# Second layer of a retention-and-MoE kernel: from eight block products to Strassen's seven

## The reference

```python
scores = scale * np.matmul(q, k.transpose(0, 1, 3, 2))   # 4 batches, 8 heads, 576 tokens, 64 dims
x = np.matmul(scores * Dmat, v)                          # decayed causal mask
h = x @ w_in                                             # first layer, 512 -> 2048
g = np.where(h >= 1, h, np.where(h <= -1, 0, (h + 1) ** 2 / 4))
x = g @ w_out                                            # 2048 -> 512
a, b = x @ w_a, x @ w_b                                  # second layer, 512 -> 1536 twice
out = (a * b) @ w_out2                                   # 1536 -> 512
```

## Time and profile before

| | |
|---|---|
| median of three runs | 913.02 us |
| the profiled execution | 915.21 us |
| its span in the trace | 912.7 us |
| TensorE busy | 902.3 us, 99% |
| VectorE, ScalarE busy | 348.2 us, 285.0 us |
| second layer on TensorE | from 462.3 us to 908.3 us |

### The profile page before, as it was taken

The page is one execution under the profiler, slowest core; times in us unless marked ns, Lnnn a source line. Parts: engine busy times, 40 slices in busy tenths (PEclk is TensorE's granted clock), DMA queues, the critical chain, the costliest instruction groups (busy, mean ns, idle before and its releaser), DMA issues.

```text
span 912.7 us, 12087 instructions
## 1 busy us (share of the span) xinstructions
PE 902.3 (99%) x5160; PEld 766.0 (84%) x5160; DVE 348.2 (38%) x565; ACT 285.0 (31%) x476; POOL 36.7 (4%) x54
## 2 busy tenths in 40 slices
PE   7999999999999999999999999999999999999998
PEld 6998888888899888888888888888899888888886
DVE  4686655434445433546653213111222311131112
ACT  1245454333445333535542112111211211121111
POOL 4550000000000000000000000000000000000000
PEclk9999999999999999999999999999999999999999
DMA  9996000000000000013330000100010000010001
GB/s 344 313 357 236 1 0 1 1 1 1 1 1 1 1 1 1 1 69 105 104 104 1 0 1 10 38 1 0 1 47 2 24 0 1 1 47 0 1 1 46
DMA packets 20053, 42.46 MB, mean 47 GB/s; under 512 B 1568, under 2 KB 12320, under 8 KB 20000
## 3 DMA queue, kind: packets, MB, share of 16 engines
q1 hardware_dynamic: 19856, 41.50, 13.1%
q10 hardware_dynamic: 144, 0.20, 0.1%
HBM read 36.97 MB, written 4.72 MB: 46 GB/s over the span
## 4 chain that ended last, share of the span: by engine, by line
PE 98%; DMA 1%; DVE 0%; ACT 0%; POOL 0%; issue 0%; SPq 0%; POOLq 0%
PE score_b L386 5%; PE score_a L386 5%; PE score_b L385 5%; PE score_a L385 5%; PE score_a L384 5%; PE score_b L384 5%; PE score_a L332 4%; PE kv_b L349 4%; PE score_a L333 4%; PE kv_b L350 4%; PE score_b L333 4%; PE score_a L334 4%; PE ret_b L350 4%; PE score_b L332 4%; PE ret_b L349 4%; PE ret_b L351 4%
## 5 line engine op out<-in xcount | busy, mean ns | idle before, releaser
L501 DVE TENSOR_TENSOR gate_w<-relu_s,relu_r 128x512 f32<-128x512 f32 (+1 forms) x80 | 51.1, 639 | 131.6 <-ACT relu_r L613 131.6
L385 PE MATMUL score_b<-xl,w_all 128*128 128x512 f32 (+1 forms) x240 | 88.3, 368 | 0.0
L386 PE MATMUL score_b<-xh,w_all 128*128 128x512 f32 (+1 forms) x240 | 88.3, 368 | 0.0
L385 PE MATMUL score_a<-xl,w_all 128*128 128x512 f32 (+1 forms) x240 | 88.3, 368 | 0.0
L386 PE MATMUL score_a<-xh,w_all 128*128 128x512 f32 (+1 forms) x240 | 88.3, 368 | 0.0
L384 PE MATMUL score_a<-xh,w_all 128*128 128x512 f32 (+1 forms) x240 | 88.2, 368 | 0.0
L384 PE MATMUL score_b<-xh,w_all 128*128 128x512 f32 (+1 forms) x240 | 88.2, 368 | 0.0
L622 ACT ACTIVATE gh<-gated 128x512 fp32r<-128x512 f32 (+1 forms) x80 | 47.2, 590 | 105.0 <-DVE gated L504 105.0
L530 DVE TENSOR_TENSOR gated<-score_a,relu_s 128x512 f32<-128x512 f32 (+1 forms) x30 | 19.1, 638 | 156.9 <-ACT relu_s L642 156.9
L510 DVE TENSOR_TENSOR gl<-gated,gh 128x512 fp32r<-128x512 f32 (+1 forms) x80 | 51.1, 638 | 50.8 <-ACT gh L622 50.6
L530 DVE TENSOR_TENSOR gated<-score_b,relu_s 128x512 f32<-128x512 f32 (+1 forms) x30 | 19.1, 637 | 126.6 <-ACT relu_s L642 126.6
(11 more groups left out here) (107 smaller groups left out, 1930.4 us busy)
## 6 DMA issues: line engine op xcount, KB each, us to landing
kq<-k_q SPq DMA_DIRECT2D x16, 576.0 KB, 6.4
w_raw<-w SPq DMA_DIRECT2D x12, 768.0 KB, 4.2
kvt<-kv_tok SPq DMA_DIRECT2D x16, 512.0 KB, 5.7
w1a_raw<-w SPq DMA_DIRECT2D x10, 512.0 KB, 9.8
out<-x_all SPq DMA_DIRECT2D x18, 256.0 KB, 3.0
w1b_raw<-w SPq DMA_DIRECT2D x6, 512.0 KB, 5.8
decays<-decays_c SPq DMA_DIRECT2D x3, 193.5 KB, 6.7
vtail<-v_tail SPq DMA_DIRECT2D x16, 32.0 KB, 5.5
```

Source lines behind the costliest of these rows:

```text
L385: pe.matmul(o, w2_slab(f, 0)[:, at], xl[:, k, 0:WIDTHS[t]], start=False, stop=False)
L386: mm = pe.matmul(o, w2_slab(f, 1)[:, at], xh[:, k, 0:WIDTHS[t]], start=False, stop=(k == KT - 1))
L501: nc.vector.tensor_tensor(gate_w[:, 0:WIDTHS[t]], relu_s[:, 0:WIDTHS[t]], relu_r[:, 0:WIDTHS[t]], ALU.add).then_inc(gatew_ready, 1)
```

## The change

The second layer is computed by Strassen's scheme in Winograd's form. The four feature tiles of x are halved into two pairs, and the tokens of a tile into two halves of 384; the two matrices a and b are the other side. Instead of the 8 block products of two feature pairs, two matrices and two token halves, there are 7 products, P1 to P7, of sums and differences of blocks.

- The tiles are now 3 of 768 tokens, with 12 blocks each: 36 steps. A step has 7 products x 2 feature tiles x 3 matmuls = 42 matmuls of 384 columns. They add in place in four PSUM banks: P1, P6 and then P7 and P4 in `main_b`, P2 in `p2_b`, P5 and P3 in `p5_b`.
- The weight operands are made during the first layer: VectorE forms four sums per block (`block_sums`), ScalarE rounds 7 operands and VectorE subtracts (`round_ops`, `split_ops`). They are stored to a tensor in memory, `w2_ops`, of 1.835 MB a block, and read back one step at a time into three buffers `wop` (`load_ops`), for each of the three tiles again.
- The token operands are made by `round_op`, `split_op` and `difference`, in the last blocks of the first layer for the first tile, and around the change of tile for the others.
- Outputs are taken over groups of four blocks: 6 rows of 128 tokens, each row in two halves of 6 matmuls of 512 columns. A step runs three such halves, 18 matmuls, from step 5 on, in one row between P7 and P5. A group's row is copied into `x_all` by ScalarE (the first group of a tile, `copy_rows`) or added there by VectorE (`add_rows`).
- The output weights of a group (4 blocks, 1 MB) are loaded into one of two buffers `wo_raw` by `load_out`, which waits until the outputs of the group before last are done (`rows_done`).

```diff
-def place2(f):
-    return NF2 - 1 if f == 0 else f - 1
-def covered1(f):
-    return min((2 * W2 * (place2(f) + 1) - 1) // (2 * W1), NF1 - 1)
+HALF = 384
+SUPER = 2 * HALF
+NS = TOK // SUPER
+ROWS = SUPER // P
+AW = 2 * P
+OPS = 7
+WOP = OPS * AW
+XBUF = 8
+WBUF = 3
+GBUF = 8
+GROUP = 4
+LAG = 5
+STEPS2 = NS * NF2
...
+        def slots(step):
+            if step < STEPS2 + 1:
+                mine = range(3 * (step - LAG), 3 * (step - LAG) + 3)
+                return [(v // 2, v % 2) for v in mine if v >= 0]
+            end = ROWS * (STEPS2 // GROUP - 1)
+            return [(end + a, h) for h in range(2) for a in range(4)] + \
+                   [(end + a, h) for a in range(4, ROWS) for h in range(2)]
...
+        prep_steps = {(1, 1): 0, (1, 5): 1, (1, 9): 2, (1, 13): 3, (2, 2): 4, (2, 8): 5,
+                      (3, 1): 6, (3, 5): 7, (3, 9): 8, (3, 13): 9, (4, 1): 10, (4, 5): 11}
...
-            def load_w2(f):
-                sp.dma_start(w2_raw(f), w2[f]).then_inc(w2_loaded[f], 16)
+            def load_ab(f):
+                if f:
+                    sp.wait_ge(op_lo_ready, 2 * f - 1)
+                sp.dma_start(ab_raw[:, :], w2_ab[f]).then_inc(ab_loaded, 16)
+            def store_ops(f):
+                sp.wait_ge(op_lo_ready, 2 * f + 2)
+                sp.dma_start(w2_ops[f, :, 0, :], raw(op_hi[:, :])).then_inc(op_stored, 16)
+                sp.dma_start(w2_ops[f, :, 1, :], raw(op_lo[:, :])).then_inc(op_stored, 16)
+            def load_ops(u):
+                if u < WBUF:
+                    end = XBUF * 2 * SUPER + 2 * WOP * (u + 1)
+                    sp.wait_ge(y_done, NF1 * (NT - 1) + (end - 1) // (2 * W1) + 1)
+                else:
+                    sp.wait_ge(p4_done, u - WBUF + 1)
+                sp.wait_ge(op_stored, 32 * (u % NF2 + 1))
+                sp.dma_start(raw(wop[u % WBUF][:, :, :]), w2_ops[u % NF2]).then_inc(wop_loaded[u % WBUF], 16)
+            def load_out(q):
+                if q < 2:
+                    sp.wait_ge(h_ready, NF1 * NT)
+                    sp.wait_ge(y_done, NF1 * NT)
+                else:
+                    sp.wait_ge(rows_done, ROWS * (q - 1))
+                at = (q * GROUP) % NF2
+                sp.dma_start(wo_raw[q % 2][:, :, :],
+                             w2_out[at:at + GROUP].rearrange("f p c -> p f c")).then_inc(wo_loaded[q % 2], 16)
...
+            for u in range(WBUF, STEPS2):
+                load_ops(u)
+                if u % GROUP == 0 and u >= 2 * GROUP:
+                    load_out(u // GROUP)
+                if u % NF2 == NF2 - 1 and u > NF2:
+                    store_rows(u // NF2 - 1)
+            store_rows(NS - 1)
...
+            def product(p, u, o, start):
+                j = u // NF2
+                if u % NF2 == 0:
+                    pe.wait_ge(xop_ready, OPS * j + X_AT[p] + 1)
+                w, b = wop[u % WBUF], x_buffer(j, X_AT[p])
+                for k in range(2):
+                    at = slice(W_AT[p] * AW + k * P, W_AT[p] * AW + (k + 1) * P)
+                    pe.matmul(o, w[:, 0, at], xop_hi[b][:, k, :], start=(start and k == 0), stop=False,
+                              skip_group_check=True)
+                    pe.matmul(o, w[:, 0, at], xop_lo[b][:, k, :], start=False, stop=False,
+                              skip_group_check=True)
+                    mm = pe.matmul(o, w[:, 1, at], xop_hi[b][:, k, :], start=False, stop=(k == 1),
+                                   skip_group_check=True)
+                return mm
...
+            def step2(u):
+                mine = slots(u)
+                if u < STEPS2:
+                    if u < 2:
+                        pe.wait_ge(relu_ready, 2 * (NF1 * NT - 3 + 2 * u))
+                    else:
+                        pe.wait_ge(prod0_ready, u - 1)
+                    pe.wait_ge(wop_loaded[u % WBUF], 16 * (u // WBUF + 1))
+                    product(1, u, main_b[u % 2], True).then_inc(p1_done, 1)
+                    if u == 0:
+                        pe.wait_ge(relu_ready, 2 * (NF1 * NT - 2))
+                    else:
+                        pe.wait_ge(a0_ready, u)
+                    product(2, u, p2_b, True).then_inc(p2_done, 1)
+                if u == 0:
+                    project(NT - 1, NF1 - 1)
+                else:
+                    pe.wait_ge(u2_copied, u)
+                    product(7, u - 1, main_b[(u - 1) % 2], False).then_inc(p7_done, 1)
+                for n, half in mine:
+                    rows(n, half)
+                if u < STEPS2:
+                    if u == 0:
+                        pe.wait_ge(relu_ready, 2 * NF1 * NT)
+                    else:
+                        pe.wait_ge(a1_ready, u)
+                    product(5, u, p5_b, True).then_inc(p5_done, 1)
+                if u:
+                    pe.wait_ge(b1_ready, u)
+                    product(4, u - 1, main_b[(u - 1) % 2], False).then_inc(p4_done, 1)
+                if u < STEPS2:
+                    pe.wait_ge(u1_copied, u + 1)
+                    product(6, u, main_b[u % 2], False).then_inc(p6_done, 1)
+                    pe.wait_ge(p5_copied, u + 1)
+                    product(3, u, p5_b, False).then_inc(p3_done, 1)
```

More of the change, by code:

```diff
@@ L410, in _ @@
-            products(0, 0)
-            project(NT - 1, NF1 - 1)
-            for u in range(1, NF2 * NT):
-                products(u // NF2, u % NF2)
-                outputs((u - 1) // NF2, (u - 1) % NF2)
-            outputs(NT - 1, NF2 - 1)
-        def o_count(t, f, a):
-            before = sum(NF2 - 1 + w // P for w in WIDTHS[:t])
-            return before + (f + 1 if f < NF2 - 1 else NF2 - 1 + a + 1)
-        w2_steps1 = {1: 0, 6: 1, 8: 2, 9: 3, 10: 4, 12: 5, 13: 6, 15: 7}
-        w2_steps2 = {0: 8, 2: 9, 3: 10, 4: 11}
+            def product(p, u, o, start):
[12 more added lines that the diff above has]
+                return mm
@@ new lines, in rows @@
+            def rows(n, half):
+                q, a = n // ROWS, n % ROWS
+                last = GROUP * q + 2 * half + 1
+                pe.wait_ge(pl_ready, 2 * last + 2)
+                pe.wait_ge(wo_ready, last + 1)
+                if n < 4:
+                    pe.wait_ge(y_copied, KT * NT)
+                elif half == 0:
+                    pe.wait_ge(rows_out[n % 4], n // 4)
+                o = y_b[n % 4]
+                for u in (last - 1, last):
+                    hi = ph[u % GBUF][:, a * P:(a + 1) * P]
+                    lo = pl[u % GBUF][:, a * P:(a + 1) * P]
+                    w_hi, w_lo = wo_hi[q % 2][:, u % GROUP, :], wo_lo[q % 2][:, u % GROUP, :]
+                    pe.matmul(o, hi, w_hi, start=(u % GROUP == 0), stop=False)
+                    pe.matmul(o, hi, w_lo, start=False, stop=False)
+                    mm = pe.matmul(o, lo, w_hi, start=False, stop=(u % GROUP == GROUP - 1))
+                if half == 1:
+                    mm.then_inc(rows_done, 1)
@@ L427, in _ @@
+            for u in range(STEPS2 + 1):
+                step2(u)
+            for n, half in slots(STEPS2 + 1):
+                rows(n, half)
         @block.vector
@@ new lines, in split_out, with add_rows @@
+            def split_out(u):
+                dve.wait_ge(wo_hi_ready, u + 1)
+                at = (u // GROUP) % 2
+                nc.vector.tensor_tensor(wo_lo[at][:, u % GROUP, :], wo_raw[at][:, u % GROUP, :],
+                                        raw(wo_hi[at][:, u % GROUP, :]), ALU.subtract).then_inc(wo_ready, 1)
+            def add_rows(step, place):
+                for n in shares_ended(step, place):
+                    if not first_share(n):
+                        dve.wait_ge(rows_done, n + 1)
+                        nc.vector.tensor_tensor(o_rows(n), y_b[n % 4].rearrange("p (k i) -> p k i", k=KT),
+                                                o_rows(n), ALU.add).then_inc(rows_out[n % 4], 1)
@@ L556, in _ @@
+            for u in range(STEPS2 + 1):
+                step2(u)
+            add_rows(STEPS2, 2)
+            for place in range(2 * ROWS):
+                add_rows(STEPS2 + 1, place)
         @block.scalar
@@ L670, in constants @@
+            for u in range(STEPS2 + 1):
+                step2(u)
+            copy_rows(STEPS2, 2)
 def constants():
@@ L711 @@
         "w1": np.concatenate([columns(moe_w_in), rows(moe_w_out)], axis=2),
[L712 removed]
+        "w2_ab": np.concatenate([columns(moe2_w_a), columns(moe2_w_b)[:, :, 2 * P:],
+                                 columns(moe2_w_b)[:, :, :2 * P]], axis=2),
+        "w2_out": rows(moe2_w_out),
         "decays_c": constants(),
```

450 lines of the change are left out of this document (291 added, 159 removed).

## The result

The changed kernel takes 943.12 us (median of four runs, 942.93 to 944.06) against 913.13 us before (median of four; 913.02 was that of three): a ratio of 1.0329, 95% interval 1.0311 to 1.0347, slower by 30 us. The forecast was 927 us, slower by 14. The direction and the mechanism were right; the slowdown was half of what came.

A forecast was written before the change was run, and what follows sets the result against it. TensorE, busy 99% of the span, was taken to bound the kernel. Terms of -34.2, +0.6, +37.1 and +10.5 summed to +14.0 us, giving 927 us by the median, range 913 to 948.

The forecast's parts named there:

- term 3: Seven TensorE gaps of 5.3 us, steps 9 to 33, operand load queued behind output load's rows_done wait: +37.1 us.
- term 4: TensorE's slower clock after each of the seven gaps, taken at 1.5 us a gap: +10.5 us (0 to 31).
- Term 1: TensorE's work in the second layer, 443.0 us before, 408.8 us after, 384-column matmuls at 173.2 ns: -34.2 us.
- R5: Rival: VectorE and ScalarE handshakes bound every second-layer step, 1 us more a step, 963 us; chance 0.06.
- Term 2: Second layer's step handshakes: covered, except P3 waiting about 0.6 us in step 1 for the P5 copy: +0.6 us.
- The first layer's additions: VectorE's sums and subtractions for 12 operand sets in the first layer, fitting its idle time: 0, bounds 0 and +3.
- the two bounds: Bounds on the seven gaps: +19.5 us if only the operand load is waited for, +48 at 340 GB/s.
- the start's 4.4: Kernel's start: after 5.88 us idle, TensorE ran 8.8 us at the lower clock, costing 4.4 us; a gap's upper price.
- R1: Rival: the seven gaps come but TensorE's clock holds, 916.5 us; chance 0.18.
- R2: Rival: each of the seven gaps pays the whole 4.4 us of slow clock, 947 us; chance 0.07.
- R3: Rival: operand load not held up by the outputs' load, 2.8 us a gap, no clock loss, 899 us; chance 0.06.
- R4: Rival: the queue's wait is hidden wholly and the change does what it says, 879.4 us; chance 0.05.

The follow-up runs named there:

- run 1: Changed kernel with a group's output-weight load issued behind step 4q+1's operand load instead of ahead of it; 881.7 us, ratio 0.9652.
- run 5: Changed kernel with output weights laid out so a partition reads one run of 8 KB instead of four of 2 KB; 935.25 us, ratio 1.0241.
- 4: Changed kernel with the row of 18 output matmuls between P2 and P7 instead of between P7 and P5; 940.95 us, ratio 1.0297.
- run 3: Changed kernel plus 26 matmuls with overwritten results before the wait for wop in the seven steps; 929.07 us, ratio 1.0177.
- run 2: Changed kernel with the rows_done wait still ahead of step 4q+1's operand load, but the output load issued behind that load; 914.23 us, ratio 1.0011.
- 6: Changed kernel with one block of four of the output load ahead of step 4q+1's operand load, three behind it; 921.86 us, ratio 1.0090.
- 7: Changed kernel with a step's three output half rows spread: one behind P7, one behind P4, one behind P3; 968.12 us, ratio 1.0597.
- 10: Changed kernel with the output load behind step 4q+1's operand load and laid out in 8 KB runs; 881.85 us, ratio 0.9652.

## Why the prediction was wrong in size

Two terms of the sum were too small: the length of a gap (term 3, 37.1 us for 43.2) and above all the slow clock behind it (term 4, 10.5 us for 18.5).

**Term 1, the work, -34.2 us: right.** The starts of the 384-column matmuls in the changed kernel are 0.173 us apart (542.26 to 544.34 holds 12), the interpolated value. The kernel without gaps (run 1) is 31.8 us faster than before; terms 1 and 2 together said 33.6. The second layer's first product starts at 461.1 us there and its last output matmul at 875.56, 414.7 us with its own stream, against 408.8 of products and outputs, 2.7 of the first layer's rest and 0.7 of waits. The difference of 2.5 is in distances that are 10 to 20 ns longer here and there. R5 (handshakes in every step) did not come.

**Term 2, the handshakes, +0.6: right.** Two short waits are left in the changed kernel, for the P5 copy and for a u copy:

```profile
PEld score_b L518 <- ACT p L948: 0.4, 1, 0.4
PEld score_b L518 <- ACT u L958: 0.3, 1, 0.3
```

The first, at 475.8 us, is P3's wait for the P5 copy in step 1, as worked out. **The first layer's additions, 0: right.** The layer's windows show VectorE at 215.81 of 362 us and TensorE without a gap:

```profile
100.00:462.00 362.00, 361.96 (x1779) 307.75 (x1778) 215.81 (x336) 172.17 (x284) 0.00 (x0) 1.00 0.24 93
```

**Term 3, seven gaps of 5.3 us, +37.1: the mechanism and the count were right, the size 6.1 us too small.** The pair landed 10.1 us after the first issue (540.52 to 550.6), not 9.2. The rate of 420 GB/s came from loads in runs of 4 KB, and the output load has runs of 2 KB. Run 5 shows that 2 KB runs instead of 8 KB cost 5.6 of the 6.1; runs of 4 KB were not tried. The measured 43.2 lies between the two bounds, +19.5 and +48. The limit of about 358 GB/s of the Trainium skill, DMA: Bandwidth & Descriptors, section on bandwidth, was quoted beside this term as one for any core; the section says that it is each core's part when both cores of an HBM domain stream. The gap shows 444 GB/s (the windows from 547.40), with this kernel on one core. That the 45 us which the limit gives came near is chance, since the time was lost at the start of the pair and not at its rate.

**Term 4, the clock, +10.5: this is the step that failed most.** The price of a gap was set at 1.5 us, a third of the start's 4.4, on the argument that the work behind a gap is dense while the start had pauses. It was 2.4 to 2.9, 18.5 in all. The start had hardly any pauses, by this window of the kernel before, the stretch that the 4.4 us come from:

```profile
5.88:14.80 8.92, 8.79 (x92) 7.85 (x92) 5.09 (x14) 0.00 (x0) 4.93 (x7) 1.00 1.04 386
```

TensorE was busy for 8.79 of 8.92 us, with matmuls of 64 and 128 columns. And behind a gap dense work of 384 columns still ran 5.1 to 6.1 us at 1.2 GHz before the clock was back. The row of a short idle at 905.37 was no help either: the 0.51 us are the weight loads' idle time, and the matmul stream stood still for 0.25 us (904.89 + 0.23 to 905.37). What followed each idle stretch of TensorE in the layer, by its length (from the end of a matmul's 0.17 us to the next start):

| run | idle stretch, us | lost behind it, us |
|---|---|---|
| 4 | 1.3 to 1.6, four (for prod0) | 0.1 |
| 3, array kept busy | 1.4 to 2.5, six | 0.1 |
| 3, array kept busy | 3.0, one | 1.65 |
| 2 | 3.1 to 3.4, three | 0.1 |
| 2 | 3.1 to 3.4, four | 1.6 |
| 6 | 3.6 to 4.8, six | 1.6 |
| 4 | 4.9 to 5.0, three | 1.6 |
| 5 | 5.1 to 5.8, seven | 1.4 to 2.9 |
| 4 | 5.2, four | 2.5 to 2.8 |
| 6 | 5.5, one | 2.4 |
| changed kernel | 5.9 to 6.3, seven | 2.4 to 2.9 |
| 7 | 10.0 to 10.5, seven | 1.8 to 2.2 |

The Trainium skill, TensorE: Matmul & The Clock Gate, in its section on the HAM clock gate, says that a kernel whose matmul groups wait for DMA pays for the re-throttled clock at each group. The changed kernel bears it out at all seven gaps, with 2.6 us a gap in the mean. The prediction had quoted the rule and then priced it by a third of the only row it had.

What decides between the losses at one length of idle, 1.4 to 2.9 us in run 5 and 0.1 or 1.6 in run 2, stays open.

The two misses together are 6.1 + 8.0 = 14.1 us, and terms 1 and 2 gave 1.8 less than they were taken for (run 1): 927 + 14.1 + 1.8 = 942.9, the measured 943.1. That this closes to 0.2 us is partly luck, since the kernel before itself took 913.0 to 913.5 us beside the different runs.

R1 (the clock holds) is out: the windows show 0.50 behind the gaps, and run 3, with the clock held but for the last place, takes 929 us, not 943. R2 (4.4 each) is out too, at 2.6 us a gap. That its 947 us are nearer to the measured time than the forecast is luck: its gaps were too short and its price too high. R3 and R4 need a shorter or hidden gap: run 2 is nearest to R3 (899 us), with gaps of 3.2 us and some loss to the clock, 914 us, and run 1 is R4's, 881.7 against the 879.4 that R4 was given. They are what the change could have done with another order.

## What to carry to other kernels

On a queue that issues in program order, put a DMA with a late wait behind every DMA that is needed sooner, or on another queue; count from the waited event, not from the place in the list, how much work is left to cover what stands behind it. When a gap of several microseconds in a busy TensorE is priced, add the slow clock behind it (here 1.4 to 2.9 us behind every gap of 3.6 us or longer), and price a load by rows with the same length of run.

## What the runs showed of the hardware that was not expected

- Equal gaps need not cost the same. Of seven idle stretches of 3.1 to 3.4 us in one execution three left the clock at 1.00 and four did not, and the same kernel's ten times spread over 4.8 us, where run 1, without gaps, stays within 0.9 us in four.
- The loss behind 10 us of idle (1.8 to 2.2 us) was smaller than behind 6 us (2.4 to 2.9): the clock was back sooner after the first matmul, 3.8 to 4.6 us against 5.1 to 6.1.
- Work whose result is thrown away made the kernel 14 us faster (943.1 to 929.1), by keeping the clock.
- Four runs of 2 KB instead of one of 8 KB in each partition cost a 1 MB load 1.1 us (5.8 against 4.7 us to landing, medians of the changed kernel and run 5), and 0.5 us in the order of runs 1 and 10 (5.3 against 4.8).
- The longer runs also evened out the DMA engines: their shares of one output load ended 0.8 to 1.2 us apart with 2 KB runs and 0.3 to 0.6 us apart with 8 KB runs.
